# Natural token order in a fused attention, Fourier mixer, MLP and gated MLP kernel, with its row table gathered by the sync queue and copied by GpSimd

## What is computed

```
# 1: attention in which a query sees only the keys of its hash bucket (sign bits of 6 projections)
mask   = q_bucket[:, :, :, None] == k_bucket[:, :, None, :]
scores = where(mask, scale * q @ k.T, -1e9);  x = softmax(scores) @ v      # [2, 768, 512]
# 2: Fourier mixing over tokens and features, then an MLP of width 2048
u = x + real(fft(fft(x, axis=1), axis=2))
x = u + relu(layernorm(u) @ w_ch1) @ w_ch2
# 3: gated MLP of width 1024, whose gate is mixed over the tokens
u, v = split(gelu(x @ w_in));  v = (w_sg @ (layernorm(v) * g_ln)) + b_sg
out = x + (u * v) @ w_out
```

## Time and profile before

| | |
|---|---|
| median of 3 runs | 779.93 us (778.46 to 780.02) |
| span of the profiled execution | 777.5 us |
| TensorE busy | 764.8 us, 98% of the span, 4614 matmuls |
| VectorE, ScalarE, GpSimd busy | 52%, 36%, 26% |
| attention, Fourier stage, MLP, gated MLP | about 0 to 286, 286 to 338, 338 to 616, 616 to 777 us |

### The profile page before, as it was taken

The page is one execution under the profiler, slowest core; times in us unless marked ns, Lnnn a source line. Parts: engine busy times, 40 slices in busy tenths (PEclk is TensorE's granted clock), DMA queues, the critical chain, the costliest instruction groups (busy, mean ns, idle before and its releaser), DMA issues.

```text
span 777.5 us, 12902 instructions
## 1 busy us (share of the span) xinstructions
PE 764.8 (98%) x4614; PEld 704.1 (91%) x4614; DVE 403.3 (52%) x738; ACT 276.8 (36%) x577; POOL 201.7 (26%) x258
## 2 busy tenths in 40 slices
PE   8999999999999999999999999999999999999998
PEld 7889999999999999998999989999999887888886
DVE  7877777777776558531132214112113387337733
ACT  4456666665665533301111111111113453014401
POOL 4133233332243573377000000000013146003300
PEclk9999999999999989999999999999999999999999
DMA  5333323233221500360000000000031000010001
GB/s 116 65 86 87 85 68 84 64 79 88 70 59 29 191 1 1 102 224 1 1 0 0 0 0 1 0 0 0 1 118 59 14 1 0 25 58 0 0 13 67
DMA packets 55569, 36.14 MB, mean 46 GB/s; under 512 B 40048, under 2 KB 48240, under 8 KB 55024
## 3 DMA queue, kind: packets, MB, share of 16 engines
q1 hardware_dynamic: 52720, 26.76, 12.0%
q0 software_dynamic: 2816, 8.94, 4.4%
HBM read 27.03 MB, written 3.15 MB: 39 GB/s over the span
## 4 chain that ended last, share of the span: by engine, by line
PE 90%; DVE 7%; issue 1%; ACT 1%; POOL 1%; DVEq 0%; POOLq 0%; ACTq 0%
PE PS L579 87%; DVE mneg L1227 2%; PE PS L594 1%; DVE ops L1207 1%; DVE Z L1323 1%; PE PS L900 1%; PE PS L846 1%; PE PS L942 1%; PE PS L868 1%; DVE fold L1310 0%; DVE Y L1330 0%; DVE ops L1197 0%; DVE Y L1331 0%; DVE ops L1194 0%; POOL vr L537 0%
## 5 line engine op out<-in xcount | busy, mean ns | idle before, releaser
L579 PEld LDWEIGHTS PS<-vn,E 128*128 128x128 f32 x1152 | 140.9, 192 | 1.6 <-ACT E L1000 1.4
L579 PE MATMUL PS<-vn,E 128*128 128x65 f32 x1152 | 140.6, 271 | 1.2 <-ACT E L1000 1.2
L1413 DVE SCALAR_TENSOR_TENSOR hL<-PS,hH 128x384 fp32r<-128x384 f32 x64 | 35.7, 557 | 201.5 <-ACT hH L1123 201.5
L579 PE MATMUL PS<-ops 98*128 98x384 f32 (+1 forms) x576 | 128.3, 354 | 1.9 <-DVE mneg L1227 1.5
L1227 DVE TENSOR_REDUCE mneg<-PS 128x1 f32<-128x768 f32 x96 | 91.8, 957 | 52.2 <-PE PS L579 51.0
L1123 ACT ACTIVATE hH<-PS 128x384 fp32r<-128x384 f32 x64 | 31.5, 492 | 231.4 <-PE PS L579 231.4
L1000 ACT ACTIVATE E<-PS 128x384 f32<-128x384 f32 x192 | 83.7, 487 | 77.6 <-PE PS L579 76.2
L579 PEld LDWEIGHTS PS<-ops 98*128 98x128 f32 (+1 forms) x576 | 96.5, 190 | 4.0 <-DVE mneg L1227 2.0
L579 PE MATMUL PS<-unTH,W1L 128*128 128x384 f32 x256 | 86.4, 337 | 0.0
L579 PE MATMUL PS<-unTH,W1H 128*128 128x384 f32 x256 | 86.2, 337 | 0.0
L579 PE MATMUL PS<-unTL,W1H 128*128 128x384 f32 x256 | 85.9, 336 | 0.0
(11 more groups left out here) (177 smaller groups left out, 1315.1 us busy)
## 6 DMA issues: line engine op xcount, KB each, us to landing
ops<-ops POOLq DMA_DIRECT2D x28, 192.0 KB, 3.0
W1R<-in_moe_w_ch_dram SPq DMA_DIRECT2D x16, 256.0 KB, 2.7
W2R<-in_moe_w_ch_dram SPq DMA_DIRECT2D x4, 1024.0 KB, 6.8
qk<-in_k_dram SPq DMA_DIRECT2D x32, 96.0 KB, 2.7
qk<-in_q_dram SPq DMA_DIRECT2D x32, 96.0 KB, 2.7
vn<-in_v_dram SPq DMA_DIRECT2D x32, 96.0 KB, 2.7
out_dram<-X SPq DMA_DIRECT2D x12, 256.0 KB, 2.1
WsgR<-in_moe_w_sg_dram SPq DMA_DIRECT2D x1, 2304.0 KB, 8.2
```

The lines of the kernel that those rows point to most:

```text
L579: return pe.matmul(dst, lhs, rhs, start=start, stop=stop, **kw)
L1413: dve.scalar_tensor_tensor(M1["hL"][:, f % 2, :], PS[:, f % 2, 0:HALF], 0.0, rd(M1["hH"][:, f % 2, :]), ALU.max, ALU.subtract).then_inc(hl ...
```

## The change

Every half is laid out as token = 128c + p: natural order. The loads of q, k, v, w_sg and b_sg and the stores follow it, the stationary operand of `second_transform` and the transposes of w_sg read 128 neighbouring columns. The host tables T1 stay as they were, so their rows are gathered: SyncE's queue loads, for each of the two tables, nine pieces (42 or 43 partitions, every third one, by two runs of 388 values) into a new plain fp32 tile T1R at 187 KB, and GpSimd copies each table to its rounded tile and then issues the loads of T2, which lie partly where T1R was. z0H, z0L and flip move to 206 KB.

```diff
+TABLE_LOADS = TH * TH
 def token_tiles(ap):
-    return ap.rearrange("(a p c) n -> p a (c n)", a=2, c=TH)
+    return ap.rearrange("(t p) n -> p t n", p=P)
...
-        t2 = run(196 * KB, ("T2H", [P, 4, QD], F32R), ("T2L", [P, 4, QD], F32R),
-                 ("z0H", [P, 2, TH], F32R), ("z0L", [P, 2, TH], F32R), ("flip", [P, 1], F32))
+        t2 = run(196 * KB, ("T2H", [P, 4, QD], F32R), ("T2L", [P, 4, QD], F32R))
+        rims = run(206 * KB, ("z0H", [P, 2, TH], F32R), ("z0L", [P, 2, TH], F32R), ("flip", [P, 1], F32))
+        STAGE = 187 * KB
...
+        R0 = layout("r0", [("T1R", STAGE, [P, 2, 2, TH, 2, NTP], F32)])
...
             def load_qk(g, s):
-                                     src[g][half(a), :].rearrange("(p c) d -> p c d", c=TH)
+                                     src[g][half(a), :].rearrange("(c p) d -> p c d", c=TH)
             def load_v(g, s):
-                                 v_h[g][half(a), :].rearrange("(p c) d -> p c d", c=TH)).then_inc(v_in[s], 16)
+                                 v_h[g][half(a), :].rearrange("(c p) d -> p c d", c=TH)).then_inc(v_in[s], 16)
...
+            def load_token_table(n, source):
+                rows = source.rearrange("p (a c n) -> p a c n", a=2, c=TH)
+                for tile_of in range(TH):
+                    for c in range(TH):
+                        first = (c - P * tile_of) % TH
+                        count, row = len(range(first, P, TH)), (tile_of * P + first) // TH
+                        sp.dma_start(R0["T1R"][first::TH, n, :, tile_of, :, :].rearrange("p a s n -> p a (s n)"),
+                                     rows[row:row + count, :, c, :]).then_inc(tab1_in[n], 16)
...
 +                if not t.looped and t.it == LOOPS and t.u == 1:
+                    load_token_table(0, t1_hi)
+                    load_token_table(1, t1_lo)
...
-            sp.dma_start(M2["bsg"][:, :, :], b_sg.rearrange("(a p c) -> p a c", a=2, c=TH)).then_inc(bsg_in, 16)
+            sp.dma_start(M2["bsg"][:, :, :], b_sg.rearrange("(a c p) -> p a c", a=2, c=TH),
+                         allow_slow_non_contiguous=True).then_inc(bsg_in, 16)
-            sp.dma_start(R2["WsgR"][:, :, :].rearrange("p (a c) n -> p a (c n)", a=2),
-                         token_tiles(w_sg)).then_inc(wsg_in, 16)
+            sp.dma_start(R2["WsgR"][:, :, :], token_tiles(w_sg)).then_inc(wsg_in, 16)
-            out_v = out.rearrange("b (a p c) n -> (b a) c p n", a=2, c=TH)
+            out_v = out.rearrange("b (a c p) n -> (b a) c p n", a=2, c=TH)
...
+            def tables():
+                for n, table in enumerate((A["T1H"], A["T1L"])):
+                    pool.wait_ge(tab1_in[n], 16 * TABLE_LOADS)
+                    pool.tensor_copy(table[:, :, :, :, :], R0["T1R"][:, n, :, :, :, :]).then_inc(tab1_rdy, 1)
+                pool.wait_ge(tab1_rdy, 2)
+                for dst, src in ((A["T2H"], t2_hi), (A["T2L"], t2_lo)):
+                    pool.dma_start(dst[:, :, :].rearrange("p i n -> p (i n)"), src).then_inc(tab2_in, 16)
...
                         sum_values(t, 1)
+                if not t.looped and t.it == LOOPS and t.u == 2:
+                    tables()
                 if t.has(-1):
                     finish_head(t)
...
-                if not t.looped and t.it == LOOPS and t.u == 1:
-                    for dst, src in ((A["T1H"], t1_hi), (A["T1L"], t1_lo)):
-                        pool.dma_start(dst[:, :, :, :, :].rearrange("p a c s n -> p (a c s n)"), src).then_inc(tab1_in, 16)
-                    for dst, src in ((A["T2H"], t2_hi), (A["T2L"], t2_lo)):
-                        pool.dma_start(dst[:, :, :].rearrange("p i n -> p (i n)"), src).then_inc(tab2_in, 16)
...
-                rows = slice(c, c + TH * (P - 1) + 1, TH)
+                rows = tile(c)
-            pe.wait_ge(tab1_in, 32)
+            pe.wait_ge(tab1_rdy, 2)
...
-                    at = a * HALF + c
-                    last = pe.transpose(PS[:, 5 + n % 3, tile(c)], R2["WsgR"][:, r, at:at + TH * (P - 1) + 1:TH], ident[:, :])
+                    last = pe.transpose(PS[:, 5 + n % 3, tile(c)], R2["WsgR"][:, r, tile(a * TH + c)], ident[:, :])
```

More of the change, by code:

```diff
@@ L116, in mixer_kernel @@
                   ("MH", [P, 4, HALF], F32R), ("ML", [P, 4, HALF], F32R), ("fold2", [P, TH, DM], F32), ("Y2", [P, TH * 4 * P], F32))
-        A = layout("a", t1 + attn + t2 + [("W1H", W1H_AT, [P, FT, KT, P], F32R),
+        A = layout("a", t1 + attn + t2 + rims + [("W1H", W1H_AT, [P, FT, KT, P], F32R),
                                                     ("W1R", W1L_AT, [P, FT, KT, P], F32)])
@@ L148, in sems @@
             return [sem(n) for n in text.split()]
-        consts, zeros, pj_in, pj_hi, pj_lo, id_r, tab1_in, tab2_in = sems("consts zeros pj_in pj_hi pj_lo id_r tab1_in tab2_in")
+        consts, zeros, pj_in, pj_hi, pj_lo, id_r, tab1_rdy, tab2_in = sems(
+            "consts zeros pj_in pj_hi pj_lo id_r tab1_rdy tab2_in")
+        tab1_in = [sem(f"tab1_in{n}") for n in range(2)]
         qk_in = [[sem(f"qk_in{s}{a}") for a in range(2)] for s in range(2)]
@@ L356, in one_time @@
                                      proj.unsqueeze(1).broadcast_to([D, 2, NBITS])).then_inc(pj_in, 16)
+                if not t.looped and t.it == LOOPS and t.u == 1:
+                    load_token_table(0, t1_hi)
+                    load_token_table(1, t1_lo)
                 if t.has(1):
```

## The result

The changed kernel takes 827.48 us, the median of 4 runs (826.57 to 828.83), against 779.26 us for the kernel before in the same session (778.46 to 780.02). The ratio is 1.062, 95% interval 1.0604 to 1.0634: 48.2 us slower. The forecast was 811.6 us, 31.7 us slower; the result lies just inside the upper end of its range, 828. The profiled execution of the changed kernel took 826.57 us, its span is 824.8.

The account below looks back on a forecast made before the run. TensorE, busy 98% of the span, was taken as the bound. A 34.8 us wait at head 14 plus 3.5 of lowered clock less 6.6 of layout gain made +31.7, so 779.9 became 811.6 us, range 798 to 828.

Parts of the forecast that it names:

- upper end of its range: High end, 828 us: half of 29 us more, if the 12 loads paid 2.4 us fixed time each in line.
- the granted clock after such a wait: TensorE behind head 14's wait: one stretch at half clock, as after a 1.25 us pause, adds 3.5 us.
- One engine for 43 partitions: Table loads: 12 loads of 43 partitions run on one engine at 24 GB/s, 66.8 us; the 42s add 2.3.
- Head 14's values: Last attention round: values queued behind the table loads land at 293.7; TensorE, wanting their sum at 260.31, waits 34.8 us.
- The layout: Neighbouring columns in `second_transform` and w_sg transposes: steps fall from 0.177 to 0.118 us; gain 6.6 us, between 0 and 7.5.
- the two waits for GpSimd's remainders: First pass of the second transform: TensorE waits 0.6 and 1.4 us for folds 2 and 3; 2.2 of 4.2 us come through.
- The covers: q, k, v pieces, w_sg's shorter pieces (4 us slack) and GpSimd's copies (2.8 us each) stay hidden, cost 0.
- B: Rival: table loads spread over engines; from two engines up the wait is gone and the gain stays, 773.3 us; chance 0.12.
- D: Rival: spread loads, but GpSimd's copies slow beside VectorE or w_sg late, a small loss, some 783 us; chance 0.03.
- C: Rival: the stride does not make `second_transform` slow; 779.9 us with spread loads, chance 0.03; 818 with one engine.

Follow-up runs that it names:

- 150 products: Changed kernel with 150 unused products of the identity with itself ahead of TensorE's wait for head 14's values: 811.00 us, ratio 1.0407.
- 30 behind it: Changed kernel with 30 unused identity products (60 matmuls) right behind TensorE's wait for head 14's value sum: 815.88 us, ratio 1.0475.
- experiment 4: Changed kernel with the 18 table loads issued behind head 14's values instead of ahead of them: 813.15 us, ratio 1.0434.
- two pairs of runs: New against old token layout, once without staging (772.87 against 778.44 us), once with staging cut into 32 and 11 rows (gains 6.9 and 0.1 us set against each other).
- experiment 1: Changed kernel with each 43-row table load cut into 32 and 11 rows, 30 loads for 18: 771.53 us, ratio 0.991.
- experiment 5: Changed kernel with each 43-row table load cut into 34 and 9 rows: 788.27 us, ratio 1.0118.
- 300 products: Changed kernel with 300 unused identity products ahead of TensorE's wait for head 14's values: 838.11 us.

## Why the prediction was right, and where it was off

**Right in mechanism, 16.5 us short in size, and inside the range in part by luck.** The step that failed is the term "the granted clock after such a wait ... I add one such stretch, 3.5 us". It measured 19.1 us. The row behind it was of a stretch in which `first_transform` ran, with matmuls of 194 columns, and here too the clock came back 3.5 us into that work. The stretch behind head 14's wait has other work in it, and all through that the clock stayed low. The row was true and was taken from the wrong place. With 150 products in the wait the term vanishes, with 30 behind it it is bought off; both say that it is the clock and not, say, GpSimd's backlog. The upper end of the range doesn't hold as worked out either: half of 29 us on top of 811.6 is 826.1, not 828, and the measured 827.48 lies above that. What that end was meant for, a fixed time paid by each load, was not what came; the clock's cost filled the gap.

**One engine for 43 partitions.** Right: 22 to 26 GB/s between the humps, and one cut, 32 and 11, brings the kernel to 771.53. The forecast took 24 GB/s, and 24 were measured.

**Head 14's values.** Landing forecast 293.7, measured 294.9; wait forecast 34.8, measured 35.2. The way there was in part another. I wrote that the values would be issued at 233 and be last in an engine's line; they were issued at 281.14, since SyncE itself was held behind each load of 43; about 0.6 us an issue held only behind the loads of 42, and 0.8 for the first two. The two pictures give the same time here, but not the same remedy: everything behind the loads in SyncE's order waits, w_ch1's slice too, as experiment 4 paid for.

**Not forecast: +1.0 us ahead of the wait.** TensorE idles 0.44 us ahead of 236.70. It stands behind two transfers between the halves of the operands, which GpSimd issues at 230.8 and 231.4 as before, but which now share the DMA engines with the table loads. The DMA issues in the stretch 230 to 237 (tile, queue, count, KB each, us to landing):

```profile
ops<-ops POOLq DMA_DIRECT2D x2, 192.0 KB, 4.1
```

Before, the same two landed after 2.8 us. That the sharing is the whole of the 1.0 us was not tried by itself.

**The layout.** Forecast 6.6 of a possible 7.5. By starts in the trace 7.8, of which (6.8 - 3.5)/2 = 1.6 us lie in the clock's shorter stay at half from the start of the transform on (3.5 us instead of 6.8), which leaves 6.2; in the two pairs of runs 5.6 and 6.8. The step of `second_transform` is (362.82 - 354.38)/71 = 0.119 us, forecast 0.118, and the load of its stationary operand fell to that of a dense one. The group of its weight loads in the changed kernel:

```profile
L602 PEld LDWEIGHTS PS<-T2H,GH 128*128 128x128 f32 x24 | 4.5, 188 | 2.0 <-issue 1.4 <-DVE GL L1364 0.6
```

262 ns became 188, and the two waits for GpSimd's remainders, forecast 0.6 and 1.4 us, are there with 0.41 and 1.19. Against the sentence of the Trainium skill, page "TensorE: Matmul & The Clock Gate", section "LDWEIGHTS (loading the stationary operand)", by which only the number of columns counts, these runs show 74 of 262 ns, over a quarter of a load's time, in the stride.

**The covers.** GpSimd's copies took 2.13 us each, not 2.8. That GpSimd's backlog is done beside the two heads held only because these took 45 us; with the clock full (150 products) TensorE waited 4.03 us at their end instead of 1.25. w_sg landed 8.4 us after an issue at 623.50 and was wanted at 635.88: hidden. The loads of q, k and v land as fast as before.

**The rivals.** B had its threshold wrong: two engines remove the named wait and still end at 788, slower than before. It asked only whether the values come in time, not when GpSimd's other work, among it the 4.3 us of copies, would then fall. D named that very collision, with 783, as a case of spread loads. With loads well spread (experiment 1) the copies are done at 259.0, ahead of VectorE's folds; the collision appears at two engines. C is out: the stride was the cause.

The rule of the Trainium skill, page "DMA: Bandwidth & Descriptors", section "Why a DMA increments its semaphore by 16 and not by 1", that a transfer takes the largest number of engines, at most 16, that divides its rows, agrees with the rates here: 43 rows at 22 to 26 GB/s, 34 rows at 50, and humps of up to 230 GB/s for 42.

## What to carry to other kernels

Look at the number of rows of each DMA before its bytes: an issue that stood behind a load of 43 partitions took 5.2 us, one behind a load of 42 took 0.63, and cutting the 43s into 32 and 11 turned a loss of 48 us into a gain of 7. A load that an engine's share can't keep up with also stops the queue's own engine, so count everything issued behind it, and moving it back in the order only moves the wait. Price a pause of TensorE not by its length but by the stretch that runs behind it: look up the granted clock for that same work, and try a burst of useless products there to see what is at stake.

## What was not expected of the hardware

- An issue on SyncE is not a fixed 0.6 us. Behind a load that ran on one DMA engine it took 4.2 to 5.6 us, about as long as that engine needs for one load (5.6), whatever the rows of the issue itself.
- The granted clock stayed at 1.2 GHz for 45 us in which TensorE was busy without a gap (44.98 of 45.00 us). It came back 3.5 to 6.8 us into the first transform in the kernels where it was low there, and within 6 us under identity products.
- A pause of 2.1 us was followed by 30.7 us at the lower level, one of 1.52 us by none in the traced run of that kernel, and its next one, of 4.03 us, by 6.8 us. The length of the pause alone did not decide it.
- GpSimd and VectorE slow each other in experiment 5: beside each other a copy took 2.85 us instead of 2.13, a fold 2.76 instead of 0.96.
- A product of two plain fp32 operands runs as two matmuls; 300 products took 67 us.
